# A fused token mixer and two feed-forward layers: rounding work dealt out anew among VectorE, ScalarE and GpSimd, and another opening order

## The reference

```python
# attn: x (2, 4096, 192), weight (8, 7)
w = exp(weight - max); w = w / (sum(w) + 1e-9)            # per head, over 7 taps
out[b, s, h, :] = sum_k w[h, k] * x_pad[b, s + k, h, :]   # 8 heads of 24 channels
x = out.reshape(8192, 192)
h = x @ w_in;  g = h / (1 + exp(-h));  x = g @ w_out      # layer one, d_ff 2048
h = x @ w_in;  g = where(h > 0, h, exp(min(h, 0)) - 1);  x = g @ w_out   # layer two
```

## Time and profile before

| what | value |
|---|---|
| runs | median 1145.17 us (1144.91 to 1145.71, three runs) |
| the profiled execution | 1145.52 us, span 1143.7 us, mean granted TensorE clock 0.997 |
| TensorE busy | 1117.0 us (98%) |
| VectorE busy | 887.3 us (78%), 1054 instructions |
| ScalarE busy | 456.3 us (40%), 500 instructions |
| GpSimd busy | 87.8 us (8%), 89 instructions, all in the first fifth of the span |

### The profile page before, as it was taken

One profiled execution on the slowest core, in us unless ns is written; L12 is line 12 of the kernel. 1 busy time (PEld: TensorE's weight loads), 2 busy tenths in 40 slices (PEclk: granted clock), 3 DMA queues, 4 the chain that ended last, 5 costly groups with the idle time before them and its releaser, 6 DMA issues.

```text
span 1143.7 us, 22350 instructions
## 1 busy us (share of the span) xinstructions
PE 1117.0 (98%) x9684; PEld 1014.9 (89%) x9684; DVE 887.3 (78%) x1054; ACT 456.3 (40%) x500; POOL 87.8 (8%) x89
## 2 busy tenths in 40 slices
PE   4899999999999999999999999999999999999998
PEld 3799999999899999888788888899989999999997
DVE  6999657779978855777997875677898786577776
ACT  5334335444422334445442332544443222354543
POOL 6758200000000000000000000000000000000000
PEclk8999999999999999999999999999999999999999
DMA  4321000000110000000101000000011000000000
GB/s 146 101 60 48 18 1 1 15 15 1 34 33 20 20 1 1 1 15 15 34 1 34 20 20 1 2 1 15 15 34 34 1 1 1 1 1 15 11 6 29
DMA packets 16881, 23.56 MB, mean 21 GB/s; under 512 B 1424, under 2 KB 9616, under 8 KB 16784
## 3 DMA queue, kind: packets, MB, share of 16 engines
q1 hardware_dynamic: 16784, 22.13, 7.0%
HBM read 15.83 MB, written 6.29 MB: 19 GB/s over the span
## 4 chain that ended last, share of the span: by engine, by line
PE 85%; DVE 11%; issue 2%; ACT 1%; DMA 0%; SPq 0%; DVEq 0%; ACTq 0%
PE acc L616 44%; PE hid L600 40%; DVE mix L401 3%; DVE g L487 2%; DVE glo L463 2%; DVE g L483 1%; ACT ghi L318 1%; DVE mix L365 1%; DVE ghi L475 1%; DMA xT<-x_rows 0%; DVE tail L441 0%; PE hid L555 0%; DVE x L455 0%; DVE mix L362 0%; DVE stg L432 0%
## 5 line engine op out<-in xcount | busy, mean ns | idle before, releaser
L600 PE MATMUL hid<-x,wi 64*128 64x512 f32 x4301 | 686.6, 386 | 0.0
L600 PEld LDWEIGHTS hid<-x,wi 64*128 64x128 f32 x4301 | 527.4, 184 | 39.8
L616 PE MATMUL acc<-ghi,wo 64*128 64x512 f32 x3036 | 543.4, 386 | 0.0
L326 ACT ACTIVATE g<-hid 128x1024 f32<-128x1024 f32 x256 | 263.2, 1028 | 660.4 <-PE hid L600 619.1
L616 PE MATMUL acc<-glo,wo 64*128 64x512 f32 x2024 | 431.0, 387 | 7.2 <-DVE glo L463 3.2
L616 PEld LDWEIGHTS acc<-ghi,wo 64*128 64x128 f32 x3036 | 397.0, 184 | 27.8
L463 DVE TENSOR_TENSOR glo<-g,ghi 128x1024 fp32r<-128x1024 f32 x256 | 317.1, 1239 | 29.4 <-ACT ghi L318 27.9
L616 PEld LDWEIGHTS acc<-glo,wo 64*128 64x128 f32 x2024 | 289.7, 184 | 32.8 <-DVE glo L463 5.9
L475 DVE CAST ghi<-g 128x1024 fp32r<-128x1024 f32 x128 | 93.8, 733 | 117.6 <-ACT g L326 117.0
L483 DVE TENSOR_SCALAR g<-g 128x1024 f32<-128x1024 f32 x128 | 88.4, 691 | 97.1 <-ACT g L326 97.0
L487 DVE SCALAR_TENSOR_TENSOR g<-hid,g 128x1024 f32<-128x1024 f32 x128 | 155.7, 1216 | 0.1
(11 more groups left out here) (60 smaller groups left out, 242.6 us busy)
## 6 DMA issues: line engine op xcount, KB each, us to landing
xT<-x_rows SPq DMA_DIRECT2D x16, 518.0 KB, 4.8
stg<-w_in SPq DMA_DIRECT2D x16, 256.0 KB, 3.2
outT<-stg SPq DMA_DIRECT2D x16, 256.0 KB, 2.1
stg<-w_out SPq DMA_DIRECT2D x16, 192.0 KB, 3.3
outT<-tail SPq DMA_DIRECT2D x16, 128.0 KB, 2.3
tap<-tap_rows SPq DMA_DIRECT2D x1, 7.0 KB, 1.6
```

The costliest lines, as they stand in the source:

```text
L326: eng.activation(g[:, u % 2, :], hid[u % 2][:, :], fn).then_inc(s_fn, 1)
L600: return eng.matmul(hid[u % 2][:, t * TOK:(t + 1) * TOK], wt, mv, start=t == home and n == 0, stop=t != home and n == 3)
L616: return eng.matmul(acc[s % 2][:, bank, :], wt[rows, 2 * j + t, cols], mv, start=bool(lead) and j == 0 and n == 0, stop=not lead and j == ...
```

## The change

- **Low parts of the weights** (five subtractions a piece) go from GpSimd to VectorE, in a period of their own per piece: `low_piece_period`, 8, 11, 14, ... 29 for pieces 8 to 15. ScalarE rounds the piece one period earlier.
- **Layer one's rounding** goes from VectorE (the CAST of L475) to ScalarE, which now applies Silu to `hid` twice, once into `ghi` (rounded) and once into `g`. In layer two `ghi` and `glo` of unit u - 1 come first in period u, ahead of Exp and of the two operations on `g`.
- **Mixing.** The rest channels of a chunk are kept as two halves of 256 columns, on LOW and HIGH, so that their taps are 128x256. The 14 taps of chunks 4, 8 and 12 are spread over 31 periods, of the others over 7, of chunk 1 over 5. The high parts (one 128x512, four 64x256 with a scale) go to ScalarE, three periods before the stage; the low parts (one 128x512, two 64x256) stay on VectorE, two periods before it.
- **Evacuation** is spread over four periods, and the rounding of its rest goes to ScalarE.
- **Opening.** The load of the taps is issued by ScalarE; x is loaded in three parts, the main group first; chunk 0 is mixed by VectorE alone; the Silu table is loaded early; TensorE does 36 matmuls on zeros ahead of its work; units 0 and 1 are done together on half rows (`begin_pair`), unit 2 by `begin_third`.

```diff
+    def evac_period(s, k):
+        return NPAIR * (s + 1) + LAG + (k if s < NSTAGE - 1 else 0)
+    CONV_OPS = 2 * NTAP + 3
+    def tap_span(c):
+        end = NPAIR * stage_of(c, 0) - 3
+        if c == 1:
+            return 0, end
+        return end - (4 * NPAIR - 1 if c % GROUP == 0 else NPAIR - 1), end
+    def hi_period(c):
+        return NPAIR * stage_of(c, 0) - 3
+    def low_period(c):
+        return NPAIR * stage_of(c, 0) - 2
+    def low_piece_period(q):
+        return q - NSTG if q < NPAIR else NPAIR + 3 * (q - NPAIR)
+    def high_piece_period(q):
+        return low_piece_period(q) - 1
...
+            def conv_hi_a(c, ready):
...
+                eng.activation(x_of(0, c)[:, 0, :], mixa[:, :], ACT.Copy, scale=tstat[:, 4:5]).then_inc(s_chi, 1)
+            def conv_hi_b(c, ready):
+                eng.wait_ge(s_conv, ready)
+                for to, rows, at in [(LOW, LOW, 0), (HIGH, HIGH, HT), (HIGH, LOW, 0), (LOW, HIGH, HT)]:
+                    eng.activation(rest_hi(0, c, to)[:, at:at + HT], mixb[rows, :], ACT.Copy,
+                                   scale=tstat[rows, 5:6]).then_inc(s_chi, 1)
...
+            def x2_hi_b(s):
+                c = chunk(s)
+                eng.wait_ge(s_tail, s + 1)
+                for rows in (lo_rows(c), hi_rows(c)):
+                    eng.activation(rest_hi(1, c, rows), tail[rows, :], ACT.Copy).then_inc(s_x2hi, 1)
...
+            split_hi(0)
             eng.wait_ge(s_tap, 7)
+            conv_hi_a(0, NTAP)
+            split_hi(1)
+            conv_hi_b(0, 2 * NTAP + 1)
+            split_hi(2)
+            for q in range(NSTG, NPIECE):
+                if high_piece_period(q) < 0:
+                    split_hi(q)
+            for u in range(LAST_PERIOD + 1):
+                if 0 < u <= NUNIT and layer((u - 1) // NPAIR):
+                    gate_hi(u - 1)
                 if u < NUNIT:
                     eng.wait_ge(s_hid, u + 1)
+                    if layer(u // NPAIR) == 0:
+                        if u >= NG:
+                            eng.wait_ge(s_mm2, u - NG + 1)
+                        eng.activation(ghi[:, u % NG, :], hid[u % 2][:, :], ACT.Silu).then_inc(s_ghi1, 1)
                     if u >= 2:
                         eng.wait_ge(s_glo, u - 1)
                     fn = ACT.Exp if layer(u // NPAIR) else ACT.Silu
                     eng.activation(g[:, u % 2, :], hid[u % 2][:, :], fn).then_inc(s_fn, 1)
                 for q in range(NSTG, NPIECE):
+                    if high_piece_period(q) == u:
                         split_hi(q)
+                for c in range(1, NCHUNK):
+                    if hi_period(c) == u:
+                        conv_hi_a(c, CONV_OPS * c + 2 * NTAP - 1)
+                        conv_hi_b(c, CONV_OPS * c + 2 * NTAP)
                 for s in range(NSTAGE):
+                    if evac_period(s, 0) == u:
+                        swap_rest(s)
+                    if layer(s) == 0 and evac_period(s, 1) == u:
+                        x2_hi_a(s)
+                    if layer(s) == 0 and evac_period(s, 2) == u:
+                        x2_hi_b(s)
...
+            def conv_low_b(c):
+                to = x_of(0, c)[lo_rows(c), 2, :]
+                eng.wait_ge(s_chi, HI_OPS * (c + 1))
+                for rows, at in ((LOW, 0), (HIGH, HT)):
+                    eng.scalar_tensor_tensor(to[:, at:at + HT], mixb[rows, :], tstat[rows, 5:6],
+                                             rest_hi(0, c, rows)[:, at:at + HT].bitcast(F32),
+                                             ALU.mult, ALU.subtract).then_inc(s_conv, 1)
...
+            low_in_rest(0)
+            low_in_rest(1)
+            conv_low_b(0)
+            low_out(0)
...
+            for u in range(LAST_PERIOD + 1):
+                if 0 < u <= NUNIT and layer((u - 1) // NPAIR):
+                    gate_low(u - 1)
+                if u < NUNIT:
+                    if layer(u // NPAIR):
+                        elu(u)
+                    else:
+                        gate_low(u)
+                for q in range(NSTG, NPIECE):
+                    if low_piece_period(q) == u:
+                        low_in_main(q)
+                        low_in_rest(q)
+                        low_out(q)
+                for c in range(1, NCHUNK):
+                    if low_period(c) == u:
+                        conv_low_a(c)
+                        conv_low_b(c)
...
+                for c, i in taps_at(u):
+                    conv_tap(c, i)
```

More of the change, by code:

```diff
@@ L56, in mixed_two_layer_ffn @@
     NSTG = 3
+    NPIECE = 2 * NPAIR
+    LOW, HIGH = slice(0, REST), slice(REST, P)
     def layer(s):
@@ L242, in _ @@
         def _(eng):
[L243 to L249, removed]
[L250 to L267 removed]
+            eng.memset(tstat[:, 7:8], 1.0).then_inc(s_tab, 1)
         @block.scalar
@@ new lines, in _, with gate_low @@
+            conv_low_a(0)
+            low_in_main(0)
+            eng.wait_ge(s_conv, NTAP + 2)
+            tap_op(0, 1, 2)
+            low_in_main(1)
+            for k in range(3, NTAP):
+                eng.wait_ge(s_conv, NTAP + 1 + k)
+                tap_op(0, 1, k)
+            low_in_rest(0)
+            low_in_rest(1)
+            conv_low_b(0)
+            low_out(0)
+            low_in_main(2)
+            low_in_rest(2)
+            low_out(1)
+            low_out(2)
+            def gate_low(u):
+                if layer(u // NPAIR):
+                    eng.wait_ge(s_ghi2, urank(u))
+                else:
+                    eng.wait_ge(s_ghi1, urank(u))
+                    eng.wait_ge(s_fn, u + 1)
+                if u >= NG:
+                    eng.wait_ge(s_mm2, u - NG + 1)
+                eng.tensor_tensor(glo[:, u % NG, :], g[:, u % 2, :], ghi[:, u % NG, :].bitcast(F32),
+                                  ALU.subtract).then_inc(s_glo, 1)
@@ L501, in _ @@
+                    if layer(s) == 0 and evac_period(s, 3) == u:
+                        x2_low_b(s)
+                for c, i in taps_at(u):
+                    conv_tap(c, i)
         @block.tensor
@@ L527, in input_ready @@
                         eng.wait_ge(s_fn, u - 1)
+            def input_ready(u):
+                s, j = divmod(u, NPAIR)
+                l, c = layer(s), chunk(s)
+                if j == 0 and s:
+                    if l == 0:
+                        eng.wait_ge(s_conv, CONV_OPS * (c + 1))
+                    else:
+                        eng.wait_ge(s_x2hi, 2 * (c + 1))
+                        eng.wait_ge(s_x2lo, 2 * (c + 1))
+                if c == 0:
+                    eng.wait_ge(s_whi, 2 * (l * NPAIR + j) + 1)
+                hidden_free(u)
             def gate_ready(u):
@@ L605, in half_second @@
                 wt = wo[layer(s)]
-                lead = bank if rows == HIGH else 1 - bank
+                leads = (rows == LOW) == (bank == 0)
                 if bank == 0:
```

541 lines of the change are left out of this document (236 added, 305 removed).

## The result

The changed kernel takes 1152.0 us (median of four runs, 1151.82 to 1153.34) where the kernel before took 1145.34 (four runs, 1144.91 to 1145.71): a ratio of 1.0061, 95% interval 1.0043 to 1.0078. It is slower by 0.6%.

What follows compares the result with a forecast made beforehand. TensorE bounds the kernel at 4.307 us a unit, stalling when input is released over 0.52 us after the previous unit's start. 1145.52 - 8.5 + 15.6 - 4.0 - 1.0 = 1147.6 us, as median 1147.3; range 1138 to 1153.

Steps and rivals of the forecast that it cites:

- Old stalls, -8.5: At the seven layer switches: the reordering and spreading remove all 8.5 us of TensorE's stalls.
- New stalls, 15.6 foreseen: Ahead of layer-one stages after the first: inputs released over 0.52 us after the previous unit's start, 15.6 us in all.
- Together 1.5: Stalls before chunks 5, 9, 13 and 1 (0.2 each) and 4, 8, 12 (0.3 each): 1.5 us after chunk 1.
- The seven at 1.46: Chunks 3, 6, 7, 10, 11, 14, 15: ScalarE's 5.8 us period delays release, 1.46 us each, 10.2 in all.
- Chunk 2's 3.9: Before chunk 2's stage: weight piece 10 adds work on ScalarE and VectorE, release at 8.7, stall 3.9 us.
- The opening, -4.0 foreseen: Start up to unit 8: T(8) at 55.3 instead of 59.28, 4.0 us less, bounds 2 to 6.
- the taps are used long before x is there: In the opening: issuing the taps' load from ScalarE delays nothing, and the first tap starts when x lands at 4.1.
- The end, -1.0: After the last unit: L487 of unit 255 can start earlier, so TensorE goes on 1.0 us sooner.
- small operations not held: Rival on ScalarE's 64x256 operations: 0.40 us instead of 0.52, 7.0 us of stalls, 1138.5 us; chance 0.20.
- no new stalls: Rival for layer-one stages: the spread causes no stalls at all, 1131.7 us; chance 0.05.
- the opening gains nothing: Rival: ScalarE waits longer for piece 3, or the clock stays low past 31; T(8) near 58, 1150 us; chance 0.10.
- The slower one: Rival for ScalarE's period 8k-3: four 64x256 cost over 0.52 each, 1151.8 us at 0.60; chance 0.15 for 0.57 or more.

Runs made afterwards that it cites:

- experiment 1: Changed kernel with the end of a chunk's mixing, its high parts and its low parts each one period earlier: 1133.44 us, ratio 0.9893.
- experiment 2: Changed kernel with the rounding of the evacuated rest (L271) and VectorE's subtraction after it (L479) one period later: 1139.2 us, ratio 0.9945.
- Experiment 7: Kernel before with only layer two's order changed, ghi and glo of unit u - 1 ahead of Exp, min and max: 1139.87 us, ratio 0.9953.
- experiment 11: Changed kernel with mixing, high and low parts one period earlier, pieces 3 to 5 split behind first Silus, taps' load on SyncE ahead of x: 1128.9 us.
- experiment 6: Changed kernel without the 36 matmuls on zeros, nothing in their place: 1151.78 us, ratio 1.0056.
- experiment 5: Changed kernel with ScalarE splitting weight pieces 3, 4 and 5 after the Silus of units 0 and 1: 1149.87 us, ratio 1.0041.
- experiment 4: Changed kernel with 24 throwaway matmuls of 128x512 after begin_pair, between units 1 and 2: 1154.49 us, ratio 1.0077.
- Experiment 10: Changed kernel with ScalarE's four 64x256 high parts ordered by the half that they read: 1151.7 us, ratio 1.0057.

## Why the prediction was right, and by how much its terms were off

- **Sign, place and mechanism held.** The change costs time because ScalarE's period 8k-3 is overfull and nothing lies between it and the deadline. Experiments 1 and 2 show it: without the lateness 18.6 us go, without L271 12.8. The size did not hold as well: the point stood 2.0 us above the kernel before, inside the 2.3 that it called no change, and the measured difference is 6.7.
- **Old stalls, -8.5:** all gone, as the table shows. Experiment 7 shows that the order of `ghi` and `glo` carries 4.4 of it; that the spreading carries the rest was not tested by itself.
- **New stalls, 15.6 foreseen, 18.4 measured.** "Together 1.5" for chunks 4, 5, 8, 9, 12, 13 was exact in sum; TensorE's waits of 0.52 before 4, 8 and 12 and of 0.23 before 5, 9 and 13 suggest that the one kind was a tenth too small and the other a tenth too large. The seven at 1.46 sum to 11.4 instead of 10.2. Of chunk 6's 0.25, 0.11 is the chain behind the first Silu, which took 4.91 us (367.58 to 372.49) for "4.8", and 0.14 a hold that I had left out: L247 starts 1.05 after L310 in chunks 6, 10 and 14, 0.90 to 0.93 in the others. Chunk 2's 3.9 was right as a release (91.47, 8.8 after 82.67, where T(14) would be without delay) and wrong as a stall: the step "release at 8.7: 3.9" took TensorE back at full clock, while for the opening's idle time I had charged the clock. That is 1.6 us, the largest error of the sum.
- **The opening, -4.0 foreseen, -2.45 measured.** The first tap began at 4.88, not "4.1", since the taps' own load, issued first on ScalarE's queue, was reduced only at 3.86. That moved the wait for piece 3 with it: issued 18.70 for "17.5", there at 22.55 for "21.4", the first pair of Silus done at 25.56 for "24.3". T(2) is 30.37 for "29.3". The rest is chunk 1's release, 0.51 for "0.2", and 0.1 in unit 3. The step that failed is "the taps are used long before x is there": in experiment 11, with the taps' load ahead of x, the reduction starts at 2.47 and the first tap at 4.03. What the parts of the new opening are worth one by one was tested only for the zeros (experiment 6). The idle time and the low clock after it were as foreseen; with the earlier trace rows, the timeline of all engines and a window:

```profile
3.86 0.17 DVE L331 TENSOR_REDUCE tstat<-tap 128x2 f32<-128x14 f32 x1 [2.47 <-DMA tap<-tap_rows]
...
4.88 0.48 DVE L343 TENSOR_SCALAR mixa<-xa,tap 128x512 f32<-128x512 f32 x1
...
18.70 0.57 SPq L209 DMA_DIRECT2D stg<-w_in  x1
...
22.55 0.63 ACT L240 ACTIVATE wi<-stg 128x512 fp32r<-128x512 f32 x1 [4.56 <-DMA stg<-w_out]
23.09 0.51 ACT L241 ACTIVATE wo<-stg 128x384 fp32r<-128x384 f32 x1
23.62 1.02 ACT L306 ACTIVATE ghi<-hid 128x1024 fp32r<-128x1024 f32 x1
...
25.70 2.47 PE L570 MATMUL hid<-x,wi 64*128 64x512 f32 x9 [5.70 <-ACT g L310]
```

```profile
24.00:30.00 6.00, 4.24 (x18) 3.07 (x20) 4.28 (x9) 5.24 (x8) 0.00 (x0) 0.50 0.46 144
```

- **The end, -1.0:** -1.1.
- **The point was 4.7 us low**, inside the range. All of the miss is in the terms above, +2.8 and +1.5 and -0.1, and 0.5 in the median, which lies 0.13 above the profiled execution and not 0.35 below. The rivals: small operations not held fell by the 0.53 steps; "no new stalls" fell; "the opening gains nothing" fell, piece 3 landing 3.85 after its issue and the clock back by 30.4. The slower one (0.57 or more for a 64x256) fell by the same rows, at 0.53; that its 1151.8 for 0.60 is nearly the measured time is chance. The time came out slower by the forecast's own mechanism with two terms too small. Two slips changed nothing: the first rival's 7.0 of stalls give 1138.7, not 1138.5, and by the page the main group of x is 259 of the 518 KB, not 265.

## What to carry to other kernels

Ahead of a stage, write down the serial chain that releases its input and the time of its deadline; the slack is what counts, and work moved to a half-idle engine costs its full length when it lands in that chain (in experiment 1 the 183 us more on ScalarE cause no stall; in the changed kernel 1.2 us ahead of a stage cost 1.3 to 1.5). Where a wait of a matmul engine is priced, price the clock after it too. Moving a prefetch one period earlier, where its buffer is free, is the cheapest thing to try: three constants gave 18.6 us.

## What the runs showed of the hardware that I had not expected

- **The clock falls after short waits.** By TensorE's loads of weights, waits of 4.11, 3.83 and 2.96 us in the steady stretch were each followed by a stretch at 1.2 GHz, and so was one of 2.30 (experiment 5). One of 2.80 (experiment 2) and those of 1.66 to 1.82 were not. After the same wait of 4.11 the clock was low from 91.8 to 95.2 in the changed kernel and from 92.4 to 99.3 in experiment 4. In the opening, the clock fell at 17.3 in experiment 4, within the idle time of 2.83 before 18.1, and it did not fall there in the changed kernel's profile. Length alone doesn't decide it.
- **ScalarE is held by reads and writes, each memory by itself.** Experiment 10 shows that a change of the half written is enough. L247, which reads SBUF from partition 0, came 1.05 behind L310 only where ScalarE's last read of SBUF had been on HIGH (ahead of chunks 6, 10 and 14, by the L252 of the chunk before), though L310 itself reads PSUM; where that read was on LOW or on all partitions it came after 0.90 to 0.93 (ten places). The Trainium skill ("VectorE: DVE Perf Modes", Two Vector instructions with no wait between them) has such a rule, with a start remembered for each memory and for reads and writes apart, for VectorE. These rows of ScalarE agree with it.
- **A load of 7 KB took 3.1 us** from its issue by ScalarE to its landing (page, part 6), with x issued beside it. Issued by SyncE ahead of x (experiment 11) it took 1.7, and its reduction started at 2.47 instead of 3.86. Whether the queue or the company makes it slow was not separated.
